# Attention with turned probabilities made directly: one-pass maxima, fed through spare operand rows

## The reference

```python
scores = scale * np.matmul(q, k.transpose(0, 1, 3, 2))
mask = block_i >= block_j                  # blocks of 64
scores = np.where(mask, scores, -1000000000.0)
scores = scores - np.max(scores, axis=-1, keepdims=True)
attn = np.exp(scores)
attn = attn / (np.sum(attn, axis=-1, keepdims=True) + 1e-09)
return np.matmul(attn, v).astype(np.float32)
```

## Time and profile before

| | us |
|---|---|
| median of 3 executions | 1098.41 (1097.65 to 1104.26) |
| the profiled execution, its own time | 1101.08 |
| its span | 1099.2 |
| TensorE busy in the span | 1050.7 (96%) |
| VectorE, ScalarE, GpSimd busy | 469.4, 380.5, 546.6 |

### The profile page before, as it was taken

One profiled execution on the slowest core, in us unless ns is written; L12 is line 12 of the kernel. 1 busy time (PEld: TensorE's weight loads), 2 busy tenths in 40 slices (PEclk: granted clock), 3 DMA queues, 4 the chain that ended last, 5 costly groups with the idle time before them and its releaser, 6 DMA issues.

```text
span 1099.2 us, 18359 instructions
## 1 busy us (share of the span) xinstructions
PE 1050.7 (96%) x6192; PEld 950.6 (86%) x6193; DVE 469.4 (43%) x1063; ACT 380.5 (35%) x926; POOL 546.6 (50%) x400
## 2 busy tenths in 40 slices
PE   4999999998989999999999999999999999999996
PEld 3888888876888989898989888889899999999895
DVE  5878888875622333333333482323232222222221
ACT  5778777774422222222222341211111111111110
POOL 7777777760000020202020224996878787878742
PEclk8999999998999999999999999999999999999999
DMA  7865555535389010101030225563535454544303
GB/s 175 212 133 130 130 121 126 129 75 168 119 305 377 4 59 0 58 0 58 0 134 1 87 75 207 124 183 68 174 74 172 76 169 79 160 89 130 42 1 48
DMA packets 71000, 122.87 MB, mean 112 GB/s; under 512 B 8104, under 2 KB 25648, under 8 KB 70960
## 3 DMA queue, kind: packets, MB, share of 16 engines
q1 hardware_dynamic: 60712, 97.03, 29.8%
q0 software_dynamic: 9920, 24.72, 11.3%
q10 hardware_dynamic: 328, 0.59, 0.2%
HBM read 81.01 MB, written 36.59 MB: 107 GB/s over the span
## 4 chain that ended last, share of the span: by engine, by line
PE 69%; POOL 1%; issue 1%; DVE 0%; ACT 0%; POOLq 0%
PE ps_turn L1462 11%; PE ps_b L1438 10%; PE ps_x L1438 10%; PE ps_a L1515 9%; PE ps_b L1515 9%; PE ps_x L1533 9%; PE ps_small L1462 7%; PE ps_a L1418 1%; PE ps_small L1410 1%; PE ps_turn L1400 1%; POOL w_high L993 1%; POOL w_low L999 1%; POOL out L1041 0%; PE ps_small L1392 0%; POOLq L737 0%
## 5 line engine op out<-in xcount | busy, mean ns | idle before, releaser
L984 POOL DMA_INDIRECT expert_rows<-x_rows,slot_idx x36 | 41.7, 1159 | 307.2 <-DVE slot_idx L1338 298.1
L1041 POOL DMA_INDIRECT out<-y_tile,out_rows x40 | 63.3, 1583 | 76.9 <-DVE y_tile L1202 72.4
L388 ACT ACTIVATE probs<-scores,neg_max 128x128 f32<-128x128 f32 (+4 forms) x160 | 91.5, 572 | 21.1 <-DVE neg_max L312 20.6
L1071 ACT CAST xT_high<-ps_a 128x512 fp32r<-128x512 f32 x40 | 23.3, 587 | 197.1 <-PE ps_a L1418 197.1
L274 DVE TENSOR_TENSOR pT_low<-turned,pT_high 128x128 fp32r<-128x128 f32 (+4 forms) x160 | 77.9, 488 | 31.6 <-ACT pT_high L350 28.7
L312 DVE TENSOR_REDUCE neg_max<-scores 128x1 f32<-128x128 f32 (+4 forms) x160 | 85.3, 533 | 2.1 <-PE scores L442 1.9
L455 PE MATMUL turned<-ident_a,probs 128*128 128x128 f32 (+1 forms) x480 | 75.8, 267 | 8.5 <-DVE pT_low L274 8.3
L1345 DVE TENSOR_TENSOR prod<-ps_b,prod 128x384 f32<-128x384 f32 x48 | 26.7, 557 | 125.1 <-ACT prod L1139 125.1
L1438 PE MATMUL ps_b<-xT_high,w_high 128*128 128x256 f32 (+3 forms) x256 | 78.0, 305 | 2.1 <-DVE xT_low L1186 1.4
L1139 ACT COPY prod<-ps_a 128x384 f32<-128x384 f32 x48 | 23.0, 479 | 163.4 <-PE ps_b L1515 163.4
L350 ACT CAST pT_high<-turned 128x128 fp32r<-128x128 f32 (+4 forms) x160 | 67.8, 424 | 31.7 <-PE turned L455 29.4
(11 more groups left out here) (219 smaller groups left out, 3089.3 us busy)
## 6 DMA issues: line engine op xcount, KB each, us to landing
spare<-e_w SPq DMA_DIRECT2D x16, 1024.0 KB, 5.4
w_raw<-e_w SPq DMA_DIRECT2D x16, 1024.0 KB, 7.6
expert_rows<-zeros SPq DMA_DIRECT2D x8, 1290.0 KB, 15.5
ex_rows<-expert_rows SPq DMA_DIRECT2D x40, 258.0 KB, 3.7
q_raw<-qT SPq DMA_DIRECT2D x34, 288.0 KB, 4.2
k_raw<-kT SPq DMA_DIRECT2D x34, 288.0 KB, 5.6
out<-zeros SPq DMA_DIRECT2D x11, 512.0 KB, 10.2
k_again<-k_parts POOLq DMA_DIRECT2D x16, 288.0 KB, 3.1
```

What stands on the lines that cost most here:

```text
L388: nc.scalar.activation(like_scores(probs[0:R, slot, 0:W], t), tile_scores(t), ACT.Exp, bias=neg_max[0:R, t:t + 1], accum_out=row_sum[hp % ...
L1041: nc.gpsimd.indirect_dma_start(out=out, out_offset=bass.IndirectOffsetOnAxis(ap=out_rows[:, j:j + 1], axis=0), in_=y_tile[j][:], in_offset ...
```

## The change

Per pair, queries and keys are used in the other order for the probabilities. A first pass, `scores`, has queries on partitions and uses high parts alone (one matmul where there were two, 96 rows deep with the mask rows); DVE takes the maxima from it (parts "one", "two0" to "four"). `turn_max` transposes the table of maxima with five transposes. ACT copies them (`copy_max`) into spare rows 96 to 104 of `q_top`, where `k_again` holds ones in the rows that a head owns. `turned_scores` then has keys on partitions and gives scores less the maximum; its 14 tiles are handled in seven units ("first", "early0" to "late1") of 256, 512, 448 or 512 columns. ACT takes exp twice of each unit: once to SBUF, rounded, as the high part, once in place in PSUM; DVE subtracts the two for the low part. No probability is transposed. v has 64 columns of ones beside its 64 columns, so `values` (the same three products) also gives the row sums; each head has an output of its own. DVE and ACT copy these outputs to `tmp`. SP gathers the sums (two small DMAs), DVE inverts them two pairs later, SP stores them to memory and reads them back spread over 64 partitions each, and GpSimd multiplies into xT, three instructions per pair. GpSimd no longer scales q nor makes v's high part; ACT takes k's and v's casts, DVE q's. The high parts that stand in two places are copied by SP (`copy_q`, `copy_k`), and operands have three buffers. The last two pairs are normalised in `fuse_output_weights`, by GpSimd. In the order of issue TensorE mixes `scores` of pair p + 1 with `turned_scores` and `values` of p. The core of the diff:

```diff
+    BANK = {"early0": 0, "early1": 1, "second0": 2, "second1": 0, "late0": 1, "late1": 2}
+    RELEASED_BY = {"early0": ("second1", -1), "early1": ("late0", -1), "second0": ("late1", -1),
+                   "second1": ("early0", 0), "late0": ("early1", 0), "late1": ("second0", 0)}
...
+            for p in range(-2, PAIRS):
+                each(rest_q, p + 1)
+                each(rest_k, p + 2)
+                each(low_v, p + 1)
+                each(normalize, p - 2)
...
+            def take_out(n):
+                dve.wait_ge(values_done, after(n, "late1"))
+                dve.wait_ge(out_taken[0], n + 1)
+                if n >= 2:
+                    dve.wait_ge(normalized, 3 * (n - 1))
+                nc.vector.tensor_copy(tmp[n % 2][1], whole_out[1]).then_inc(out_taken[1], 1)
...
+            for p in range(-2, PAIRS + 1):
+                if p < PAIRS:
+                    each(invert, p - 2)
+                each(max_of, p + 1, "one")
+                each(low, p, "first")
+                each(take_out, p - 1)
+                each(max_of, p + 1, "two0")
+                each(max_of, p + 1, "two1")
+                each(low, p, "early0")
+                each(max_of, p + 1, "three0")
+                each(max_of, p + 1, "three1")
+                each(low, p, "early1")
+                each(max_of, p + 1, "four")
+                each(low, p, "second0")
+                each(low, p, "second1")
+                each(low, p, "late0")
+                each(cast_q, p + 2)
+                each(low, p, "late1")
 
...
+            def exps(n, unit):
+                act.wait_ge(turned_done, after(n, unit))
+                if n:
+                    act.wait_ge(values_done, after(n - 1, unit))
+                nc.scalar.activation(unit_of(pT_high, unit), unit_scores(unit), ACT.Exp, scale=SCALE).then_inc(high_done, 1)
+                nc.scalar.activation(unit_scores(unit), unit_scores(unit), ACT.Exp, scale=SCALE).then_inc(exp_done, 1)
...
+            for p in range(-1, PAIRS + 1):
+                each(take_out, p - 1)
+                each(exps, p, "first")
+                each(cast_k, p + 2)
+                each(exps, p, "early0")
+                each(exps, p, "early1")
+                each(high_v, p + 1)
+                if p < OPERANDS - 2:
+                    mask(p + 2)
+                    own(p + 2)
+                each(exps, p, "second0")
+                each(exps, p, "second1")
+                each(exps, p, "late0")
+                each(copy_max, p + 1, 0)
+                each(exps, p, "late1")
+                each(copy_max, p + 1, 1)
...
+            def scores(n, part):
...
+                if part == "two0" and n:
+                    pe.wait_ge(low_done, after(n - 1, "first"))
+                if part in ("two1", "three0", "three1", "four"):
+                    pe.wait_ge(max_found, at + {"two1": 1, "three0": 2, "three1": 3, "four": 5}[part])
+                top, again = q_top[u][0:MAX_ROW], k_again[u][0:MAX_ROW]
...
+                elif part == "four":
+                    for k in range(2):
+                        keys = slice(k * S // 2, (k + 1) * S // 2)
+                        nc.tensor.matmul(work[:, SHARED + k, 0:S // 2], top[:, 1, S - P:S], again[:, 1, keys], start=True, stop=True)
+                        nc.tensor.matmul(work[0:BLOCK, SHARED + k, 0:S // 2], top[:, 0, S - BLOCK:S], again[:, 0, keys], start=True, stop=True)
+                    for h in range(2):
+                        mm = nc.tensor.matmul(work[:, SHARED + h, S // 2:S // 2 + P], top[:, h, 0:P], again[:, h, 0:P], start=True, stop=True)
+                else:
+                    i, h = {"two": 2, "three": 3}[part[:-1]], int(part[-1])
+                    mm = nc.tensor.matmul(work[:, SHARED + h, 0:(i + 1) * P], top[:, h, i * P:(i + 1) * P], again[:, h, 0:(i + 1) * P],
+                                          start=True, stop=True)
+                mm.then_inc(scores_done, 1)
...
+            def turned_scores(n, unit):
...
+                    pe.wait_ge(q_copied[u], 16 * (n // OPERANDS + 1))
+                    pe.wait_ge(max_copied, 2 * n + 1)
...
+                else:
+                    if unit == "early0":
+                        pe.wait_ge(max_copied, 2 * n + 2)
+                    released, shift = RELEASED_BY[unit]
+                    if n + shift >= 0:
+                        pe.wait_ge(low_done, after(n + shift, released))
+                    h, out = int(unit[-1]), work[:, BANK[unit]]
+                    tiles = {"early": [(out[:, 0:LATER], h, 0, P, S), (out[:, LATER:LATER + BLOCK], h, 4, S - BLOCK, S)],
+                             "second": [(out[:, 0:LATER], h, 1, P, S)],
+                             "late": [(out[:, 0:LATER - P], h, 2, 2 * P, S), (out[:, LATER - P:2 * LATER - 3 * P], h, 3, 3 * P, S)]}[unit[:-1]]
+                for out, h, c, begin, end in tiles:
+                    keys = slice(c * P, (c + 1) * P)
+                    nc.tensor.matmul(out, k_parts[u][:, h, keys], q_mix[u][:, h, begin:end], start=True, stop=False)
+                    mm = nc.tensor.matmul(out, k_again[u][:, h, keys], q_top[u][:, h, begin:end], start=False, stop=True)
+                mm.then_inc(turned_done, 1)
...
+            for p in range(-1, PAIRS + 1):
+                each(turned_scores, p, "first")
+                each(scores, p + 1, "one")
+                each(values, p - 1, "late1")
+                each(turned_scores, p, "early0")
+                each(scores, p + 1, "two0")
+                each(scores, p + 1, "two1")
+                each(turned_scores, p, "early1")
+                each(turned_scores, p, "second0")
+                each(scores, p + 1, "three0")
+                each(values, p, "first")
+                each(scores, p + 1, "three1")
+                each(turned_scores, p, "second1")
+                each(values, p, "early0")
+                each(scores, p + 1, "four")
+                each(turned_scores, p, "late0")
+                each(values, p, "early1")
+                if p + 1 < PAIRS:
+                    turn_max(p + 1)
+                each(turned_scores, p, "late1")
+                each(values, p, "second0")
+                each(values, p, "second1")
...
+            for h in range(2):
+                pool.wait_ge(out_taken[h], PAIRS)
+                nc.gpsimd.dma_start(sums[h * D:(h + 1) * D, (PAIRS - 1) % 2], row_of_sums(tmp, PAIRS - 1, h)).then_inc(last_sums, 16)
+            store(PAIRS - 2)
+            spread(PAIRS - 2)
+            store(PAIRS - 1)
+            normalize(PAIRS - 2)
+            spread(PAIRS - 1)
+            normalize(PAIRS - 1)
...
+                if slot == PIECES - 1:
+                    dve.wait_ge(normalized, 3 * PAIRS)
```

More of the change, by code:

```diff
@@ L31, in attention @@
     SCALE = D ** -0.5
     MASKS = masks.shape[1]
[L33 to L53, removed]
@@ L56, in attention @@
-    values_at = {0: [(0, 0)], 1: [(0, 1)], 2: [(0, 2)], 3: [(0, 3), (0, 4)],
-                 5: [(1, 0)], 6: [(1, 1)], 7: [(1, 2), (1, 3), (1, 4)]}
+    MAX_ROW = 96
+    MAX_ROWS = own_rows.shape[0]
+    LATER = S - P
+    OPERANDS = 3
+    UNITS = ("first", "early0", "early1", "second0", "second1", "late0", "late1")
+    AT = {"early": 0, "second": LATER + BLOCK, "late": 2 * LATER + BLOCK}
+    WIDE = {"early": LATER + BLOCK, "second": LATER, "late": (LATER - P) + (LATER - 2 * P)}
+    AT_FIRST = sum(WIDE.values())
@@ new lines, in attention @@
+    COLUMNS = AT_FIRST + P
+    BANK = {"early0": 0, "early1": 1, "second0": 2, "second1": 0, "late0": 1, "late1": 2}
+    RELEASED_BY = {"early0": ("second1", -1), "early1": ("late0", -1), "second0": ("late1", -1),
+                   "second1": ("early0", 0), "late0": ("early1", 0), "late1": ("second0", 0)}
+    SHARED = 3
+    SCORES = ("one", "two0", "two1", "three0", "three1", "four")
+    MAXES = len(SCORES) + 1
+    SUMS_ROW = (D, 0)
+    OUT_AT = (BLOCK, 2 * 512 - P)
+    tmp, inv_rows, sums, inverses, stored = kept
@@ L78, in attention @@
[L78 to L88, removed]
@@ L333, in _, with cast_q @@
-            batches(dve, emit)
-            invert(LAST - 1)
-            for t in range(STEPS - LOW_LAG, STEPS):
-                low(LAST - 1, t)
-            take_out(LAST - 1, BATCHES - 1, PAIRS - 1)
+                nc.vector.reciprocal(inverses[:, n % 2], den[:]).then_inc(inv_ready, 1)
+            def cast_q(n):
+                dve.wait_ge(q_loaded[n % 2], 16 * (n // 2 + 1))
+                if n >= OPERANDS:
+                    dve.wait_ge(turned_done, after(n - OPERANDS, "late1"))
+                nc.vector.tensor_copy(q_top[n % OPERANDS][0:D], q_raw[n % 2][0:D]).then_inc(q_cast, 1)
@@ new lines, in take_out, with cast_k @@
+            def take_out(n):
+                act.wait_ge(values_done, after(n, "late0"))
+                if n >= 2:
+                    act.wait_ge(normalized, 3 * (n - 1))
+                nc.scalar.copy(tmp[n % 2][0], whole_out[0]).then_inc(out_taken[0], 1)
```

(15 more changed lines are left out.)

731 lines of the change are left out of this document (361 added, 370 removed).

## The result

The changed kernel took 1090.36 us (median of 9 runs, 1087.63 to 1097.2), the one before 1102.52 us on the same chip (9 runs, 1097.65 to 1104.68): a ratio of 0.990, 95% interval 0.988 to 0.993. So 1.0% was gained where 2.5% was forecast. The profiled execution took 1087.6 us (span 1085.8); the forecast for it was 1073.1.

What follows compares the result with a forecast made beforehand. TensorE was taken to bound the attention stage, at 12.3 + 0.5 = 12.8 us a pair. Profiled execution 1101.08 - 28.3 + 0.3 = 1073.1 us, median 1070.4; own range 1061 to 1081, stated range up to 1094.

Steps and rivals of the forecast that it cites:

- the cover of the loop of sums: SP's transfers of sums and inverses, priced at nothing; `normalize` was to end some 2 us before `take_out` needs it.
- Rival A: Attention pairs: handovers bind, or the loop of sums uses up its 2 us; 14.0 us a pair, 1088.4 us, chance 0.20.
- the hand-overs (a) to (c): TensorE's three tight places, "two0", "three0" and "second1", waiting for DVE's results; all claimed to hold with 0.3 us.
- place (a): `scores` "two0" behind the low part of "first": ready at 2.0 us, TensorE there at 2.3 us.
- Start of iteration 0: Masks, k's cast and copy, then the first pair's maxima and transposes: start at 21.5 us, bounds 20 to 24.
- The other fourteen: Attention pairs after the first, each taken at 12.3 + 0.5 = 12.8 us.
- The 0.05 us at each of 21 entries: TensorE's overhead on entering each group of matmuls in a pair: 1.05 us a pair.
- The new waits, 0.5: TensorE's waits per pair at the three tight places: 0.5 us taken, between 0 and 2.0.
- rival C: Attention pairs: dense waits lower TensorE's clock, costing 2.3 us more; 16.1 us a pair, 1120 us, chance 0.10.
- Last iteration and copy out: Last pair, without scores: a chain of exps, subtractions and values, 10.5 us, and copy out 1.0 us.
- The next stage: `fuse_output_weights`, with the last inversions and GpSimd's six products: 0.3 us lost, bounds 0 to 3.
- The rule of the Trainium skill: `fuse_output_weights`: GpSimd's six products, 5.5 us, would stop DVE's cuts for as long at most.

Runs made afterwards that it cites:

- experiment 1: Changed kernel without the division by row sums (no transfers of sums, no inversions, GpSimd multiplies by a constant): 1065.3 us, ratio 0.967 to the kernel before.
- Experiment 5: Changed kernel with SP issuing the loads of mask rows and `own_rows` ahead of q and k: 1084.1 us, ratio 0.983 to the kernel before.
- experiments 8 and 9: Changed kernel, prefetch in 256 KB pieces: with third buffer, early inverses, masks first 1057.3 us; third buffer, masks first 1055.9; alone 1089.8. Unsplit, third buffer, masks first: 1060.0.
- experiment 4: Changed kernel with ACT doing the exps of "first" ahead of `take_out`: 1077.1 us, ratio 0.978 to the kernel before.
- experiment 2: Changed kernel with a third buffer for the outputs (`tmp`), all work kept: 1066.0 us, ratio 0.969 to the kernel before.
- experiment 7: Changed kernel with third buffer, early inverses, masks first and exps of "first" before `take_out`: 1061.7 us; then with `take_out` first again: 1064.8 us.

## Why the prediction was half right

**The step that failed** is the cover of the loop of sums: "Their users come an iteration later (three operand buffers), so I price them at nothing ... Walked through by the order in which the diff issues, `normalize` ends some 2 us before that." In pair 3 it ended 3.2 us after ACT needed it. The operands have three buffers, `tmp` has two. The step named the right victims (GpSimd's `normalize`, through `tmp` ACT's `take_out`) and then took a margin from a walk that isn't shown. In the trace the spread is issued 5.6 us after the head of pair 2 and lands 6.6 us later, and three products take 3.03 us and not 2.75: 15.3 us from the head of the pair, which itself took 12.25. Over the program a spread needs 3.9 us to land at the median and up to 5.9. Rival A had this mechanism in half a sentence, at 0.20. Its time, 1088.4, is 2.0 us from the measured one, and that is in part luck: its pairs of 14.0 us measured 13.25 on average, and the late start and the longer stages behind fill the rest. Its other half, the hand-overs (a) to (c), is not what happened: TensorE did wait at place (a), but only because ACT's copy out was late; without the loop (experiment 1) the margins of 0.3 us held in all fourteen pairs.

**The terms**, against the forecast's 1073.1 for the profiled execution (1087.6; 14.5 us over):
- Start of iteration 0: 21.5, measured 25.39, +3.9. The 9-row load of `own_rows` was issued behind 1.2 MB of q, k and the identity (four loads of 288 KB and one of 64) and landed at 12.0 us, where the mask rows, the cast and the copy of k had been put at 12 together. Experiment 5 takes all of it back and 3 us more.
- Iteration 0: 14.45 us for 12.8, +1.7. Until 33.4 us its matmuls of 448 columns start 0.38 us apart, not 0.21, as they do in pair 3 at a granted clock of 0.50.
- The other fourteen: 13.16 us for 12.8, +5.0. This hides two errors against each other. The 0.05 us at each of 21 entries, 1.05 a pair, isn't there: 11.23 us is the raw sum. The new waits, 0.5, are 1.9 with what followed them, 27.0 us in fourteen pairs: 15.6 us of idle time at "two0", 9.4 us of slower matmuls in pairs 3 and 10, where the wait (2.7 and 1.7 us) was followed by the lower clock, and 2.0 us more. The slower matmuls are rival C's mechanism, at 0.7 us a pair where it had 2.3; it didn't decide the sign.
- Last iteration and copy out: 12.35 for 11.5, +0.9.
- The next stage: 1.1 us longer than before, where 0.3 was taken and 3 was the bound, +0.8. GpSimd's products end 23.6 us into it, where some 15 had been estimated.
- Behind it 2.4 us more. In the experiments this part takes 793.1 to 796.6 us from kernel to kernel, with the same instructions; I take it for scatter, which isn't shown.

**What held:** TensorE's cadences by width, the exps' price, DVE's low parts and the balance of engines (ACT 10.1, DVE 10.0 us a pair, where 9.5 and 9.4 were summed), and so the direction. With the single buffer added the kernel takes 1066.0 us, 4.4 under the forecast. That nearness is in part errors that cancel: its fourteen pairs take 11.6 us, not 12.8, and its start and its first pair (25.4 and 15.7 us for 21.5 and 12.8) cost more.

**The rule of the Trainium skill** (SBUF — State Buffer, Who interferes with whom) that a DVE instruction with two SBUF inputs contends with a GpSimd instruction that reads SBUF, of which the prediction said that no row of the kernel before shows it, has its rows now: 2.37 us for 1.23, and 0.87 and 1.92 for 0.69, beside GpSimd's products. That is 2.5 us of DVE's time in the profiled execution, under the 5.5 us at most; what it costs TensorE isn't shown. The attention stage's subtractions, which read one input from PSUM, kept their 686 ns.

What stays open: why some pairs of the change lose nothing and others 5 to 9 us. Which pairs are long differs from kernel to kernel (pairs 3 and 10 in the change; 3, 5, 7 and 11 with the prefetch in pieces). The length of the wait alone doesn't decide it. Pairs 7, 8, 10 and 12 of the change each have one wait of 1.68 us at the same place; pair 10 took 16.2 us, the others 13.1 at a granted clock of 1.00, as pair 8 here:

```profile
133.01:146.12 13.11, 11.43 (x80) 10.91 (x78) 10.40 (x19) 10.11 (x20) 10.90 (x9) 1.00 1.00 247
```

The loop brings the waits; how much one costs goes with the clock behind it, which no experiment here varied by itself. Pair 0 took from 13.6 to 18.2 us from kernel to kernel, with the same work on TensorE; this too was not settled.

## What to carry to other kernels

A step "off the critical path" has to be followed through every buffer that it frees: count the buffers of each tile in the loop, not those of the operands beside it, and give the transfer its longest landing in the trace, not the median. When a loop through a DMA closes within two iterations, a third buffer costs 4.6 KB per partition here (2 x 576 values) and gave 2.2% of the kernel, in the total as much as removing the loop. Small transfers on which a stage's start hangs are issued first (experiment 5), and once the loop has slack, large prefetches on the same queue are cut into pieces (experiments 8 and 9).

## What the hardware showed unexpectedly

- A wait can cost more than itself: 2.74 us of TensorE's idle time in pair 3 was followed by matmuls of 448 columns at 0.38 us apart, and the pair was 9.0 us longer. It need not be that long: in experiment 4 a wait of 1.14 us stood before 6.8 us at a granted clock of 0.50, and the pair took 16.4 us. In experiment 2, with waits up to 1.3 us, no pair after the first took over 12.7.
- In the first pair the matmuls run at the rate that pair 3 has at a granted clock of 0.50, 1.2 GHz (448 columns 0.38 us apart at 27 us, 0.2 from 33.7 us on), while the granted clock of the same stretch reads 1.00. The column doesn't show every slow stretch; the cadence does.
- Exps that write PSUM take as long as those that write SBUF: 601 and 603 ns for 512 columns.
- Transfers of 2.2 KB behind a prefetch of 1 MB and some loads of k took up to 8.3, 7.3 and 8.6 us from issue to landing (both kernels of experiment 7, and third buffer and masks alone), where the medians are 3.9 to 4.3; with the prefetch cut up none took over 5.9 and the long pair went from 16.8 to 12.1 us. In the change none took over 5.9 with the 1 MB loads either, so the size alone doesn't make them late.
- DVE subtractions with both inputs in SBUF took 2.37 us for 1.23 and 1.92 for 0.69 beside GpSimd's products.
